# Log-decay sums in four quarters, a scan that returns scaled states, and r and k loaded without padding rows

## What is computed

```python
for t in range(S):
    cur = einsum('bhd,bhe->bhde', u * k[t], v[t])
    y[t] = einsum('bhd,bhde->bhe', r[t], state + cur)
    state = w[t][..., None] * state + einsum('bhd,bhe->bhde', k[t], v[t])
# then: logits = x @ phi; softmax over tokens and over slots, 8 experts of 4 slots; h = x @ w_in; g = h * sigmoid(1.702 h); g @ w_out
```

## Time and profile before

| what | us |
|---|---|
| median of three runs | 400.38 |
| the profiled execution's own time | 400.66 |
| its span | 398.9 |
| PE busy / DVE / ACT / POOL | 390.8 / 242.9 / 187.7 / 49.0 |
| attention, first logarithm to last y transpose | 3.9 to 135.9 |
| five scaling copies on ACT, 16 pairs | 23.5 |
| logarithm sums on PE, 192 records | 25.7 |

### The profile page before, as it was taken

One profiled execution on the slowest core, in us unless ns is written; L12 is line 12 of the kernel. 1 busy time (PEld: TensorE's weight loads), 2 busy tenths in 40 slices (PEclk: granted clock), 3 DMA queues, 4 the chain that ended last, 5 costly groups with the idle time before them and its releaser, 6 DMA issues.

```text
span 398.9 us, 8722 instructions
## 1 busy us (share of the span) xinstructions
PE 390.8 (98%) x3290; PEld 312.0 (78%) x3290; DVE 242.9 (61%) x453; ACT 187.7 (47%) x418; POOL 49.0 (12%) x50
## 2 busy tenths in 40 slices
PE   7998999999999999999999999999999999999996
PEld 6887888888888743458888888888888888888885
DVE  4888886978788765257765454454545545455451
ACT  4787887878787523065443222422332242223221
POOL 3532442235223200000000000000000000000000
PEclk9999999999999999999999999999999999999999
DMA  8999999999999899930000100200020020002002
GB/s 288 391 359 395 371 362 364 321 354 392 326 364 362 352 424 398 411 163 2 1 2 31 48 2 0 80 0 1 0 79 0 0 79 2 0 2 79 0 2 79
DMA packets 15859, 68.66 MB, mean 172 GB/s; under 512 B 1744, under 2 KB 2896, under 8 KB 14800
## 3 DMA queue, kind: packets, MB, share of 16 engines
q1 hardware_dynamic: 15824, 68.18, 44.5%
HBM read 63.46 MB, written 4.72 MB: 171 GB/s over the span
## 4 chain that ended last, share of the span: by engine, by line
PE 94%; DMA 2%; DVE 1%; issue 1%; ACT 1%; POOL 0%; ACTq 0%; DVEq 0%; SPq 0%; POOLq 0%
PE bank L1231 32%; PE bank L1235 16%; PE bank L1010 6%; PE bank L897 6%; PE bank L1202 6%; PE bank L1041 5%; PE bank L1033 3%; PE bank L1131 3%; PE bank L1151 3%; PE bank L992 2%; PE bank L977 2%; DMA nat<-nat_in 2%; PE bank L956 1%; PE bank L917 1%; PE bank L936 1%; PE bank L894 1%
## 5 line engine op out<-in xcount | busy, mean ns | idle before, releaser
L628 ACT ACTIVATE ring<-bank 128x512 f32<-128x512 f32 x96 | 57.3, 598 | 138.4 <-PE bank L1202 138.3
L866 DVE CAST g_split<-ring 128x512 fp32r<-128x512 f32 x96 | 41.0, 427 | 88.2 <-ACT ring L628 88.2
L1231 PE MATMUL bank<-g_split,wo_hi 128*128 128x512 f32 x285 | 80.1, 389 | 0.0
L1231 PE MATMUL bank<-g_split,wo_lo 128*128 128x512 f32 x285 | 80.0, 389 | 0.0
L1235 PE MATMUL bank<-g_split,wo_hi 128*128 128x512 f32 x285 | 80.0, 389 | 0.0
L868 DVE TENSOR_TENSOR g_split<-ring,g_split 128x512 fp32r<-128x512 f32 x96 | 66.5, 693 | 3.3
L1231 PEld LDWEIGHTS bank<-g_split,wo_lo 128*128 128x128 f32 x285 | 53.5, 188 | 11.1
L1235 PEld LDWEIGHTS bank<-g_split,wo_hi 128*128 128x128 f32 x285 | 53.5, 188 | 11.1
L1231 PEld LDWEIGHTS bank<-g_split,wo_hi 128*128 128x128 f32 x285 | 53.4, 188 | 11.2 <-DVE g_split L866 0.2
L1202 PE MATMUL bank<-cst,mst 128*128 (+1 forms) x96 | 37.4, 391 | 0.0
L446 POOL TENSOR_TENSOR nat<-nat 128x576 f32<-128x576 f32 x16 | 22.6, 1412 | 79.9 <-DMA nat<-nat_in 33.9
(11 more groups left out here) (162 smaller groups left out, 424.9 us busy)
## 6 DMA issues: line engine op xcount, KB each, us to landing
nat<-nat_in SPq DMA_DIRECT2D x32, 576.0 KB, 6.5
rk<-rk_in SPq DMA_DIRECT2D x16, 768.0 KB, 6.5
ring<-w_in SPq DMA_DIRECT2D x16, 768.0 KB, 8.1
w2a<-w_in SPq DMA_DIRECT2D x4, 1536.0 KB, 7.4
out_t<-ring SPq DMA_DIRECT2D x5, 768.0 KB, 3.5
ring<-w_in SPq DMA_DIRECT2D x6, 512.0 KB, 6.8
ring<-win_in SPq DMA_DIRECT2D x3, 1024.0 KB, 7.8
ring<-wout_in SPq DMA_DIRECT2D x4, 768.0 KB, 13.4
```

Source lines behind the costliest of these rows:

```text
L628: a.activation(gact[:, s % NG, :], bank[6 + s % 2][:, :], ACT.Gelu_apprx_sigmoid).then_inc(g_done, 1)
L866: v.tensor_copy(g_hi[:, s % NG, :], gact[:, s % NG, :]).then_inc(ghi_done, 1)
L1231: t.matmul(bank[3 * par + o][:, :], wo[:, f, P * o:P * (o + 1)], g_hi[:, s % NG, :], start=(f == 0 and wo is wo_hi), stop=False)
```

## The change

Each chunk's logarithm sum is made in four quarters (64 tokens by one head), for the tokens before the middle into one bank and for those after it into another; the middle column of `pinv` and `pw` is set to 1 once. The scan adds first and multiplies second, over six columns a channel with a zero factor in the sixth, and writes `sc` itself; `scaled_states` and its semaphore go. Its 288 columns in bank 5 reach into the place of the slot logits, which move to the last 128 columns of banks 6 and 7. r and k of pairs 2 to 15 come from an array without padding, as two transfers of 48 partitions. Three warm-up calls write to bank 4.

```diff
...
         rk, nat = (rk0, rk1), (nat0, nat1)
-        tsum = sb(gen1, "tsum", [P, D * (NC - 1)])
-        frep = sb(gen1, "frep", [P, D * (NC - 1)])
-        sc = sb(gen1, "sc", [P, NC - 1, D])
+        sc = sb(gen1, "sc", [P, D, NC])
+        frep = sb(gen1, "frep", [P, D, NC])
         fdec = sb(gen1, "fdec", [P, NC - 1])
...
             def load_rk(n, slot, used=None):
-                if used is not None:
-                    sp.wait_ge(inter_done, used)
-                sp.dma_start(rk[slot][:, :, :], rk_in[bass.ds(n, 1)].rearrange("a p q t -> (a p) q t")).then_inc(ld_rk[slot], 16)
+                if used is None:
+                    sp.dma_start(rk[slot][:, :, :], rk_in[n]).then_inc(ld_rk[slot], 16)
+                    return
+                sp.wait_ge(inter_done, used)
+                for h in range(HP):
+                    sp.dma_start(rk[slot][HOFF * h:HOFF * h + D, :, :],
+                                 rk_more[bass.ds(n - 2, 1), h].rearrange("a e q t -> (a e) q t")).then_inc(ld_rk[slot], 16)
...
-            src = [bank[q][0:DP, 0:G3 * (P + 1)].rearrange("p (c t) -> p c t", c=G3) for q in range(2)]
+            src = [bank[half][0:DP, 0:NC * MID].rearrange("p (c t) -> p c t", c=NC) for half in range(2)]
+            tokens = [slice((MID + 1) * half, (MID + 1) * half + MID) for half in range(2)]
...
                     act.wait_ge(logsum_done if q else first_logsums, 1)
-                    a.activation(pinv[0:DP, chunks, :], src[q], ACT.Exp, scale=-1.0).then_inc(inv_done, 1)
-                    a.activation(pw[0:DP, chunks, :], src[q], ACT.Exp).then_inc(exp_done, 1)
+                    sums2 = [bank[2 * q + half][0:DP, 0:G3 * MID].rearrange("p (c t) -> p c t", c=G3) for half in range(2)]
+                    for half in range(2):
+                        ins = a.activation(pinv[0:DP, chunks, tokens[half]], sums2[half], ACT.Exp, scale=-1.0)
+                    ins.then_inc(inv_done, 1)
+                    for half in range(2):
+                        ins = a.activation(pw[0:DP, chunks, tokens[half]], sums2[half], ACT.Exp)
+                    ins.then_inc(exp_done, 1)
...
                 for q in range(2):
-                    a.activation(pinv[0:DP, G3 * q:G3 * (q + 1), :], src[q], ACT.Exp, scale=-1.0).then_inc(inv_done, 1)
+                    a.activation(pinv[0:DP, :, tokens[q]], src[q], ACT.Exp, scale=-1.0).then_inc(inv_done, 1)
                 for q in range(2):
-                    a.activation(pw[0:DP, G3 * q:G3 * (q + 1), :], src[q], ACT.Exp).then_inc(exp_done, 1)
+                    a.activation(pw[0:DP, :, tokens[q]], src[q], ACT.Exp).then_inc(exp_done, 1)
...
                     act.wait_ge(state_done, s.i)
-                a.activation(frep[0:DP, :].rearrange("p (e c) -> p c e", e=D)[:, 1:NC - 1, :],
-                             fdec[0:DP, 0:NC - 2].unsqueeze(2).to_broadcast([DP, NC - 2, D]), ACT.Copy).then_inc(frep_done, 1)
-            def scaled_states(s):
-                act.wait_ge(state_done, s.i + 1)
-                if not s.first:
-                    act.wait_ge(inter_done, s.i)
-                for c in range(NC - 1):
-                    ins = a.activation(sc[0:DP, c, :], tsum[0:DP, :].rearrange("p (e c) -> p e c", e=D)[:, :, c], ACT.Copy, scale=fdec[0:DP, c:c + 1])
-                ins.then_inc(scaled, 1)
+                a.activation(frep[0:DP, :, :].rearrange("p e c -> p c e")[:, 0:NC - 1, :],
+                             fdec[0:DP, :].unsqueeze(2).to_broadcast([DP, NC - 1, D]), ACT.Copy).then_inc(frep_done, 1)
...
                 a.activation(lgT[0:G3 * NS, :], src, ACT.Copy).then_inc(lgt_out, 1)
+            def lgt_evacuate_beside_y(b):
+                act.wait_ge(lgt_done, b + 2)
+                act.wait_ge(logit_done, b + 1)
+                for j in range(2):
+                    ins = a.activation(lgT[0:G3 * NS, P * j:P * (j + 1)], bank[6 + j][0:G3 * NS, BANK - P:BANK], ACT.Copy)
+                ins.then_inc(lgt_out, 1)
...
                 r, k = rk[s.slot][0:DP, 0, :], rk[s.slot][0:DP, 1, :]
-                dve.wait_ge(ld_rk[s.slot], 16 * s.loads + 16)
+                dve.wait_ge(ld_rk[s.slot], 16 * HP * s.loads + 16)
                 dve.wait_ge(inv_done, 2 * s.i + 2)
...
                 v.tensor_tensor(r3, r3, pw[0:DP, :, 0:P], ALU.mult).then_inc(rc_done, 1)
-                dve.wait_ge(scaled, s.i)
+                dve.wait_ge(frep_done, s.i)
                 v.tensor_tensor(fdec[0:DP, :], pw[0:DP, 0:NC - 1, P], pinv[0:DP, 1:NC, 0], ALU.mult).then_inc(f_done, 1)
...
                 if not s.first:
-                    dve.wait_ge(scaled, s.i)
-                v.tensor_tensor_scan(tsum[0:DP, :], frep[0:DP, :], bank[5][0:DP, 0:D * (NC - 1)], 0.0,
-                                     ALU.mult, ALU.add).then_inc(state_done, 1)
+                    dve.wait_ge(inter_done, s.i)
+                v.tensor_tensor_scan(sc[0:DP, :, :].rearrange("p e c -> p (e c)"), bank[5][0:DP, 0:D * NC],
+                                     frep[0:DP, :, :].rearrange("p e c -> p (e c)"), 0.0, ALU.add, ALU.mult).then_inc(state_done, 1)
                 if not s.first:
...
-            def log_sum(c):
-                return t.matmul(bank[c // G3][0:DP, (c % G3) * (P + 1):(c % G3 + 1) * (P + 1)], lw[:, c, 0:DP], tri[:, :],
-                                start=True, stop=True)
+            def log_sum(c, banks, col):
+                for half in range(2):
+                    rows = slice(MID * half, MID * (half + 1))
+                    for h in range(HP):
+                        ch = slice(HOFF * h, HOFF if h == 0 else DP)
+                        ins = t.matmul(bank[banks[half]][ch, MID * col:MID * (col + 1)], lw[rows, c, ch],
+                                       tri[rows, (MID + 1) * half:(MID + 1) * half + MID], start=True, stop=True)
+                return ins
...
                         pe.wait_ge(ln_done if c else first_ln, 1)
-                    ins = log_sum(c)
+                    ins = log_sum(c, (2 * (c // G3), 2 * (c // G3) + 1), c % G3)
                     if c == G3 - 1:
...
                 for c in range(NC):
-                    ins = log_sum(c)
+                    ins = log_sum(c, (0, 1), c)
                 ins.then_inc(logsum_done, 1)
...
                     slot_logits_part(dst, m)
+            def slot_logits_beside_y():
+                for m in range(CM):
+                    for j in range(2):
+                        for g in range(G3):
+                            ins = t.matmul(bank[6 + j][NS * g:NS * (g + 1), BANK - P:BANK], phi[:, m, :], xT[:, m, 2 * g + j, :],
+                                           start=(m == 0), stop=(m == CM - 1))
+                ins.then_inc(lgt_done, 1)
...
                     for h in range(HP):
-                        ins = t.matmul(bank[5][HOFF * h:HOFF * h + D, 0:D * (NC - 1)].rearrange("p (e c) -> p e c", e=D)[:, :, c], kcn[:, c, HOFF * h:HOFF * h + D],
+                        ins = t.matmul(bank[5][HOFF * h:HOFF * h + D, 0:D * NC].rearrange("p (e c) -> p e c", e=D)[:, :, c], kcn[:, c, HOFF * h:HOFF * h + D],
                                        nat[s.slot][:, 0, HD * c + D * h:HD * c + D * (h + 1)], start=True, stop=True)
...
                     pe.wait_ge(ld_phi, 16)
-                    pe.wait_ge(state_done, s.i + 1)
-                    slot_logits(bank[5][:, LOGIT:LOGIT + 2 * P])
+                    pe.wait_ge(x_done, 2 * s.i)
+                    slot_logits_beside_y()
                 if n1 is not None:
...
                     pe.wait_ge(x_done, 2 * s.i)
+                if xg == G3 and n1 is not None:
+                    pe.wait_ge(lgt_out, b + 1)
                 if n1 is None:
...
                     early_transposes(bank[1], 2)
-                pe.wait_ge(scaled, s.i + 1)
+                pe.wait_ge(state_done, s.i + 1)
                 for c in range(1, NC):
...
                         rows, half = slice(HOFF * h, HOFF * h + D), half_of(h, c)
-                        ins = t.matmul(bank[6 + c % 2][half:half + D, P * (c // 2):P * (c // 2 + 1)], sc[rows, c - 1, :],
+                        ins = t.matmul(bank[6 + c % 2][half:half + D, P * (c // 2):P * (c // 2 + 1)], sc[rows, :, c - 1],
                                        r[rows, P * c:P * (c + 1)], start=(c <= 2), stop=False, skip_group_check=True)
...
     arrays = {
-        "rk_in": np.ascontiguousarray(np.stack([channels_first(r), channels_first(k)], axis=2)),
+        "rk_in": np.ascontiguousarray(np.stack([channels_first(r), channels_first(k)], axis=2)[0:2]),
+        "rk_more": np.ascontiguousarray(np.stack([a.reshape(pairs, 2, S, D).transpose(0, 1, 3, 2) for a in (r, k)], axis=3)[2:]),
         "w0_in": tokens_first(w)[0],
...
```

More of the change, by code:

```diff
@@ L14, with decay_attention_soft_moe_gelu_kernel @@
 BANK = 512
-def decay_attention_soft_moe_gelu_kernel(nc, rk_in, w0_in, nat_in, u_in, phi_in, w1_in, w2_in, win_in, wout_in, out_t):
-    PAIRS, _, _, S = rk_in.shape
```

(19 more changed lines are left out.)

## The result

The kernel after takes **431.13 us** (428.01 to 432.11, four runs) beside 400.7 for the kernel before on the same chip: a ratio of 1.0753, with a 95% interval of 1.0692 to 1.0814. Forecast were 395.3 us and a range of 391.5 to 404. The profiled execution has a span of 429.3 us (398.9 before) and took 431.06. First the page of the changed kernel: busy time, the slices for clock and DMA, the DMA queues, the chain that ended last and the DMA issues.

What follows compares the result with a forecast made beforehand. The prediction took PE to set the pace, with the DMA close behind. Its terms -5.5-0.2+0.9+0.5-0.8 = -5.1 us gave 395.3 us against the median of 400.38, with a range of 391.5 to 404.

Steps and rivals of the forecast that it cites:

- What bounds the kernel: Attention part: PE sets the pace at 8.08 us a pair; the DMA, needing 7.3 us, follows with under 10% to spare.
- Part 4: Unpadded r and k loads in 14 pairs: fewer bytes shorten waits for data, -0.8 us, if both transfers take under 2.15 us.
- the upper end of 4.0: Load of r and k: highest cost considered for the two transfers, each as dear as one of 128 partitions, 4.0 us.
- The gain of -0.8: Shorter waits for data before the updates and the logarithms, from unpadded r and k: -0.8 us in total.
- Narrow transfers: Rival at r and k's load: 48 partitions at half rate, 3.0 us; decides from 2.15, loss past 2.7; 405 us, chance 0.16.
- Part 1: Logarithm sums in quarters: 48 records at 23.8 ns, 1.14 us instead of 1.51, in 15 pairs: -5.5 us.
- Quarters at full speed: Rival at the logarithm sums: 15 ns a record, another 0.4 us a pair, 391.5 us; chance 0.09.
- The rule of 25 ns: PE's logarithm sums: matmuls never start closer than about 25 ns, so sums take 1.20 us and the saving is 0.31.
- Part 2: Scan that scales, without ACT's five copies: scan 0.78 us, weights read with a step; +0.9 us from pairs 4, 8, 12.
- strided weights: Inter-chunk products reading sc in steps of 24 bytes: taken as free; rival doubles records, +9.8 us, 405, chance 0.06.
- The +0.9 for the starts of batches: Pairs 4, 8 and 12: longer scan makes DVE late with the second mask, 0.3 us each, +0.9 us.
- Part 3: Slot logits beside y in pairs 7 and 11: 36 records, same 1.50 us, plus waiting for x_out: +0.5 us for both.

Runs made afterwards that it cites:

- e2: Kernel before with r and k of the later pairs brought as two transfers of 48 partitions, nothing else changed: 422.55 us, ratio 1.0457.
- e11: Kernel before with 192 KB a pair less, still on all 128 partitions (part of tokens-first r not loaded): 399.93 us, ratio 0.9994.
- e8: Kernel before, r and k from the third pair on as one transfer of 112 partitions: 420.23 us, ratio 1.0436.
- e7: Kernel before with only the logarithm sums in quarters (48 records a pair) and their Exp: 407.02 us, ratio 1.0155.
- e1: Changed kernel with the old load of r and k, padded, one transfer of 128 partitions: 410.37 us, ratio 1.0226.
- e13: e1 with 21 warm-up products of 256 columns written as four of 64 each, 63 more PE records: 407.45 us, ratio 1.0145.
- e5: e1 with the old logarithm sums (12 records a pair) and their Exp: 402.01 us, ratio 1.0011.
- e9: e1 with the 14 later loads of the first weights moved behind the attention part: 419.68 us.
- e10: Kernel before with the 14 later loads of the first weights moved behind the attention part: 417.2 us.
- e6: e1 with the logarithm sums as products of 64 rows by 112 columns, 24 records a pair instead of 48: 402.63 us, ratio 1.0014.

## Why the prediction was wrong

The sign was wrong, and the size by 36 us. By the steps of the text:

**What bounds the kernel.** Right as it was read: PE sets the pace, the DMA follows "with under 10% to spare". But a margin of 0.7 us a pair called for care with each term that touches the DMA, and the forecast spent it on its likeliest case.

**Part 4, the first step that failed.** "I take a value below that, because the bytes are the only thing the rows price": under 2.15 us for the two transfers. The runs give 3.7 us for 112 rows and 4.9 for twice 64. For twice 48, e2's ratio gives +18 us in 14 pairs, 1.3 us a pair over 8.08, so 9.4 us of DMA less 5.3: some 4.1 us, just past the upper end of 4.0 that I had. The end was there; by the rule used for the other terms (between ends far apart, the row it is nearest to) bytes were not nearer than the untested width. The gain of -0.8 was nothing as well (e11).

**The rival "Narrow transfers".** The right mechanism with the right place and turning point, at 0.16 too rare and at 3.0 us too cheap: it gave 405. With 4.0 it would have given (9.3-8.08) x 14 = 17 us more, 417, close to what e2's ratio gives. What it took from the Trainium skill, SBUF — State Buffer, was borne out in the direction: 48 and 64 rows are slow here and two such transfers don't make up for it. The reason given there in section "Door 1", the ports reached, would not have foreseen e8, where 112 rows cost as much.

**Part 1, the second step that failed.** The term for PE's time was mis-sized the other way: 0.72 us instead of 1.14, since (0.92-0.23)/47 = 14.6 ns a record (mean length 232 ns), the rival "Quarters at full speed". The rule of 25 ns that spoke against this part (the Trainium skill, TensorE: Matmul & The Clock Gate, section "Wait — 56ns, not 53.3ns?") does not hold for these products. What was **missing** is a term for the instructions themselves: 48 records instead of 12 make PE's program of a pair a third longer, its pieces come too late, and PE stands. e7 prices the part at +6.2 us where I had -5.5. In e1 the sums save 15 x 0.79 = 11.9 us, the six stops at borders are 14.8 us long together, and its granted clock is at the lower level, 1.2 GHz, for 14 us, up to 7 us of work lost: +9.9. That profile's execution took 413.54 us, 12 more than the kernel before, so some 2 us of it stay open. No rival held this.

**Part 2.** Right: scan 0.76 for 0.78, strided weights 0.04 us a pair (0.83 from start to start in e13's rows above, 0.79 before), and e5's total is neutral. The +0.9 for the starts of batches shows once the sums are short: pairs 8 and 12 of e9 gain 0.16 us on e10 where the sums alone would give 0.79, so some 0.6 is lost in each where I had 0.3; pair 4 loses next to nothing (7.08 against 7.73). **Part 3.** Right: pairs 7 and 11 take 9.13 and 9.08 us in e5 and 8.89 and 8.79 before, 0.5 us for both, with 36 records in 1.51 us and 0.22 of waiting for x_out in pair 7.

**The sum.** -5.1 us was to come out of terms of at most 5.5; e2 and e1 give +18 and +9, and the whole is +30. That the two add up rather than overlap fits what the rows show, that they are felt at different moments, the waits for w and v between groups and the stops mostly within them; no run tests it.

No version of the change that was tried beats the kernel before: the nearest, e5 and e6, are the same within their intervals.

## What to carry to other kernels

Keep loads into SBUF on all 128 partitions when the DMA has little to spare: a quarter of padding was free here, and bringing r and k without it took about twice the DMA time (an estimate of 3.7 to 4.1 us against 2.0). Count PE's instructions along with its columns: cutting products into quarters made this group twice as fast and a pair's program a third longer, and the stops cost more than the time saved. When a step has one end of its cost past the point at which it decides, the forecast's likeliest case should not be the cheap one for want of a row.

## What was not expected of the hardware

- A transfer of 112 partitions, 672 KB, cost as much of the kernel's time as two of 48 (ratios 1.0436 and 1.0457, against 1.0009 for two of 128).
- Products of 64 rows, 64 or 48 weight columns and 64 moving columns in four quarters start every 14.6 ns; as row halves with 112 columns they take about 52 ns.
- PE stands 1.3 to 3.3 us (e1, e7, e13) at single borders of 16 KB in its program when it goes through them faster and the DMA is full, until 1.2 to 1.5 us after the piece has landed; and the products behind some of the stops run at the lower clock for a stretch: 15 records in 1.94 us at 24.30 us of the kernel after, where 24 take 1.52. The row, and the stretch behind it with its granted clock of 0.50:

```profile
24.30 1.94 PE L1067 MATMUL bank<-at,nat 128*48 128x128 f32 x15 [3.67 <-issue]
```

```profile
24.30:28.40 4.10, 4.10 (x26) 3.45 (x25) 1.59 (x4) 2.17 (x5) 0.00 (x0) 0.50 1.07 229
```
